# Weaving the next block's first products into the last steps of a block, in an attention and two-layer gated kernel on one Trainium2 core

## The chip, the cores and the metric

The kernel runs on one core of a Trainium2 chip. A core has TensorE (PE in the profile, with its weight loads as PEld), VectorE (DVE), ScalarE (ACT), GpSimd (POOL) and SyncE (SP, which issues the DMAs). The metric is the device time of one execution in microseconds, lower is better. Inputs and outputs lie in HBM in fp32; a difference in time of about 0.5% is what a measurement of this kernel can tell from no change.

## The reference

Pooled attention is followed by two gated two-matrix layers over the same 4608 tokens of width 512, with 2048 hidden features.

```python
def _attn_ref(q, k, v):                       # q, k, v: (8, 8, 576, 64)
    k_p = k.reshape(B, H, Sp, 8, D).mean(axis=3)
    v_p = v.reshape(B, H, Sp, 8, D).mean(axis=3)
    scores = scale * np.matmul(q, k_p.transpose(0, 1, 3, 2))
    scores = scores - np.max(scores, axis=-1, keepdims=True)
    attn = np.exp(scores)
    attn = attn / (np.sum(attn, axis=-1, keepdims=True) + 1e-09)
    return np.matmul(attn, v_p)

def _moe_ref(x, w_in, w_out):                 # layer 1
    h = x @ w_in
    g = np.where(h >= 1, h, np.where(h <= -1, 0.0, (h + 1) ** 2 / 4.0))
    return g @ w_out

def _moe2_ref(x, w_in, w_out):                # layer 2
    h = x @ w_in
    g = h - np.tanh(h)
    return g @ w_out
```

## The kernel before, in words

Everything is kept feature-major: a tile holds 128 features on its partitions and tokens along its columns. Layer 1 works through 16 blocks of 288 tokens (blk 0 to 15, two per batch entry), layer 2 through 9 blocks of 512 tokens. The attention of the next block runs inside the current layer 1 block. Every operand of TensorE is split in two (hi and lo, fp32r), and each product is the sum of three: hi times hi, hi times lo, lo times hi.

A block has FT = 16 hidden tiles of 128 features. For hidden tile j:

- `first_product(j)` on TensorE is 4 x 3 = 12 matmuls into one PSUM bank, the bank that `h_bank(j)` names. Its end increments `h_done`.
- In layer 1 the gate is a chain of five instructions: `clip` (DVE, L822), `bend` (ACT, the square, L678), `gate1` (DVE, maximum, L828), `round_gate` (ACT, g_hi, L687) and `split_gate` (DVE, g_lo, L815), which increments `g_split`. In layer 2 there is no clip: `bend` is a tanh from PSUM (L682), then `gate2` (L834), `round_gate` (L689), `split_gate` (L812).
- `second_product(j)` on TensorE is again 12 matmuls, three into each of the four banks of `acc_ps`, which are summed over the 16 tiles. The last one into each bank increments `acc_done`.

PSUM has eight banks of 512 fp32 columns: two in `h_ps`, `score_ps`, `att_ps`, and four in `acc_ps`. In layer 1 the first products alternate between the two banks of `h_ps`, but tile 2 goes into `att_ps`. In layer 2 four banks are used in turn.

The order of the work is written out by hand for each engine, as a loop over steps s = 0 to 15 of a block (`block_body`), and each engine runs its own list in order. On TensorE, step s is `second_product(s)`, then `first_product(s + 3)` as long as that tile is in the block (LAG = 3), with pieces of the next block's attention between them. So steps 13, 14 and 15 hold only second products. They are followed by the first products of tiles 0, 1 and 2 of the next block (written f0', f1', f2' below), and then by a wait for the sums to be read out of `acc_ps`, before second_product(0) of the next block may overwrite them.

DVE in step s does `split_gate` of tile s + 1 and then the clip and gate of tile s + 2; ACT does `round_gate` of tile s + 1 and `bend` of tile s + 2. The read-out, `copy_sums`, is two copies on ACT (L701, banks 0 and 2) and two on DVE (L842, banks 1 and 3); both engines have it in step 14, ahead of the clip or bend of tile 16, which is tile 0 of the next block.

DVE has work of the next batch entry too: `pool_k` (L853), the pooling of k, is one reduction in each of steps 11 to 14 of the blocks 0, 2, ... 12; sum_v, place_v and split_v stand in steps 0 to 7 of the blocks 1, 3, ... 13. Block 15 is the switch: its tiles are of layer 1, but f0', f1' and f2' after it are of layer 2, and the weights of layer 2 are loaded and split in it.

## Time and profile before

| | |
|---|---|
| median of 3 runs | 1795.99 us (1793.92 to 1802.9) |
| the profiled execution | 1793.92 us |
| its span, first to last instruction | 1792.0 us |
| PE busy | 1738.9 us (97%), 10480 matmuls |
| PEld busy | 1577.8 us (88%) |
| DVE busy | 874.3 us (49%) |
| ACT busy | 546.9 us (31%) |
| mean granted TensorE clock | 0.992 of full speed |
| chain that ended last | PE 85%, DVE 11%, ACT 2% |

The span is cut into two parts by the layers: up to about 985 us the layer 1 blocks, from there to the end the layer 2 blocks. In a timeline row the first number is the start in us, the second the duration in us, then engine, line, operation and tiles; a bracket holds the time for which the engine had been idle before the row, and what released it. Successive matmuls overlap in the pipeline, so the distance from one start to the next (0.13 us for 288 columns) is what a matmul costs, not its duration (0.29 us).

### The profile page before, as it was taken

What the parts mean: (1) busy time and instruction counts of PE and PEld (TensorE: products, weight loads), DVE (VectorE), ACT (ScalarE), POOL (GpSimd) and SP (SyncE); (2) the same over time, 40 slices, a digit from 0 to 9 for tenths busy, and PEclk for the clock granted to TensorE, in tenths of its full rate; (3) what the DMA queues carried; (4) which work ended last, traced back from release to release, by engine and by line L of the source; (5) the groups of instructions that cost most, each with busy time, mean ns of one, the idle gap of its engine ahead of it and who ended that gap; (6) DMA issues with size and microseconds to landing.
All of it is one profiled execution on the core that took longest, in us unless ns stands there. A gap on an engine that the chain in (4) does not pass through costs nothing.

```text
span 1792.0 us, 25053 instructions
## 1 busy us (share of the span) xinstructions
PE 1738.9 (97%) x10480; PEld 1577.8 (88%) x10480; DVE 874.3 (49%) x1745; ACT 546.9 (31%) x1141; POOL 160.2 (9%) x136
## 2 busy tenths in 40 slices
PE   4999999999999999999999999999999999999998
PEld 4999999999999999999999888888888888888887
DVE  6576676666856767668554222222222223232222
ACT  3533333333333333333335222222222222222221
POOL 4700011001000110011006100000000000000000
PEclk7999999999999999999999999999999999999999
DMA  5421012011110120111023101010101010000000
GB/s 163 153 63 64 15 39 77 26 30 61 39 64 16 37 78 26 58 34 39 14 71 132 60 0 48 0 47 0 47 5 42 9 38 15 32 18 29 23 1 24
DMA packets 47608, 77.81 MB, mean 43 GB/s; under 512 B 3488, under 2 KB 19872, under 8 KB 47520
## 3 DMA queue, kind: packets, MB, share of 16 engines
q1 hardware_dynamic: 47520, 76.56, 13.0%
q8 instruction: 64, 1.05, 0.2%
q14 instruction: 24, 0.20, 0.0%
HBM read 57.67 MB, written 18.87 MB: 43 GB/s over the span
## 4 chain that ended last, share of the span: by engine, by line
PE 85%; DVE 11%; ACT 2%; issue 0%; POOL 0%; DMA 0%; DVEq 0%; SPq 0%
PE acc_ps L502 40%; PE h_ps L492 29%; PE att_ps L492 6%; PE score_ps L492 6%; PE score_ps L517 2%; DVE k_diag L853 2%; DVE g_lo L815 1%; DVE v_sum L864 1%; DVE h_ps L828 1%; DVE bent L822 1%; PE score_ps L537 1%; ACT bent L678 1%; PE att_ps L529 1%; DVE v_tail L886 1%; DVE row_sum L907 1%; DVE prob L900 1%
## 5 line engine op out<-in xcount | busy, mean ns | idle before, releaser
L502 PE MATMUL acc_ps<-g_hi,wout_hi 128*128 128x288 f32 (+1 forms) x1600 | 541.0, 338 | 10.5 <-DVE g_lo L815 10.5
L502 PE MATMUL acc_ps<-g_hi,wout_lo 128*128 128x288 f32 (+1 forms) x1600 | 529.2, 331 | 0.0
L502 PE MATMUL acc_ps<-g_lo,wout_hi 128*128 128x288 f32 (+1 forms) x1600 | 528.9, 331 | 0.0
L492 PE MATMUL h_ps<-x_hi,win_hi 128*128 128x288 f32 (+1 forms) x1248 | 405.0, 325 | 15.0 <-DVE g_lo L815 9.6
L492 PE MATMUL h_ps<-x_hi,win_lo 128*128 128x288 f32 (+1 forms) x1248 | 398.6, 319 | 0.0
L492 PE MATMUL h_ps<-x_lo,win_hi 128*128 128x288 f32 (+1 forms) x1248 | 396.2, 317 | 0.0
L502 PEld LDWEIGHTS acc_ps<-g_hi,wout_hi 128*128 128x128 f32 x1600 | 302.6, 189 | 39.8 <-DVE g_lo L815 10.1
L502 PEld LDWEIGHTS acc_ps<-g_lo,wout_hi 128*128 128x128 f32 x1600 | 303.2, 190 | 25.3
L502 PEld LDWEIGHTS acc_ps<-g_hi,wout_lo 128*128 128x128 f32 x1600 | 302.4, 189 | 24.1
L492 PEld LDWEIGHTS h_ps<-x_hi,win_hi 128*128 128x128 f32 x1248 | 235.5, 189 | 31.5 <-DVE g_lo L815 13.6
L492 PEld LDWEIGHTS h_ps<-x_lo,win_hi 128*128 128x128 f32 x1248 | 237.1, 190 | 12.9
L492 PEld LDWEIGHTS h_ps<-x_hi,win_lo 128*128 128x128 f32 x1248 | 235.8, 189 | 12.8
L678 ACT ACTIVATE bent<-bent 128x288 f32<-128x288 f32 x256 | 113.9, 445 | 395.0 <-DVE bent L822 395.0
L815 DVE TENSOR_TENSOR g_lo<-h_ps,g_hi 128x288 fp32r<-128x288 f32 x240 | 109.3, 455 | 145.1 <-ACT g_hi L687 143.7
L834 DVE TENSOR_TENSOR h_ps<-h_ps,bent 128x512 f32<-128x512 f32 x72 | 50.4, 699 | 215.6 <-ACT bent L682 215.6
L828 DVE TENSOR_TENSOR h_ps<-h_ps,bent 128x288 f32<-128x288 f32 x240 | 110.6, 461 | 71.8 <-ACT bent L678 71.8
L822 DVE TENSOR_SCALAR bent<-h_ps 128x288 f32<-128x288 f32 x240 | 108.1, 450 | 59.6 <-PE h_ps L492 59.4
L682 ACT ACTIVATE bent<-h_ps 128x512 f32<-128x512 f32 x72 | 43.1, 599 | 227.8 <-PE h_ps L492 227.8
L687 ACT CAST g_hi<-h_ps 128x288 fp32r<-128x288 f32 x240 | 95.5, 398 | 39.2 <-DVE h_ps L828 39.2
L435 POOL TENSOR_TENSOR prob_tail<-prob,row_rcp 96x128 f32<-96x128 f32 x48 | 19.9, 415 | 754.4 <-DVE row_rcp L916 754.4
L834 DVE TENSOR_TENSOR att_ps<-att_ps,bent 128x512 f32<-128x512 f32 x36 | 25.2, 700 | 120.2 <-ACT bent L682 120.2
L492 PE MATMUL att_ps<-x_hi,win_lo 128*128 128x512 f32 (+1 forms) x208 | 76.1, 366 | 0.0
(125 smaller groups left out, 1825.1 us busy)
## 6 DMA issues: line engine op xcount, KB each, us to landing
stage<-kT SPq DMA_DIRECT2D x16, 576.0 KB, 5.2
q_sb<-qT SPq DMA_DIRECT2D x16, 576.0 KB, 3.9
x2T_scratch<-prob SPq DMA_DIRECT2D x16, 576.0 KB, 3.7
x_lo<-x2T_scratch SPq DMA_DIRECT2D x9, 1024.0 KB, 7.0
yT<-out_sb SPq DMA_DIRECT2D x9, 1024.0 KB, 5.0
stage<-v SPq DMA_DIRECT2D x8, 1024.0 KB, 8.3
stage<-w_in SPq DMA_DIRECT2D x8, 1024.0 KB, 5.0
stage<-w_out SPq DMA_DIRECT2D x8, 1024.0 KB, 5.3
```

Source lines behind the costliest of these rows:

```text
L435: nc.gpsimd.tensor_tensor(prob_tail[0:CH, c].rearrange("p (i a r) -> p i a r", i=2, a=PAIRS), tails.unsqueeze(1).to_broadcast(shape), seco ...
L492: last = nc.tensor.matmul(h_bank(j, layer)[:, 0:WIDTH[layer]], w[:, c, j * P:(j + 1) * P], x[:, c, 0:WIDTH[layer]], start=(c == 0 and i == ...
L502: last = nc.tensor.matmul(acc_ps[:, m, 0:WIDTH[layer]], w[:, j, m * P:(m + 1) * P], g[:, j % GRING, 0:WIDTH[layer]], start=(j == 0 and i = ...
L517: last = nc.tensor.matmul(bank[0:CH, e * 2 * KEYS:(e + 1) * 2 * KEYS], q_sb[:, p, c * CH:(c + 1) * CH], k_diag[:, p, :], start=True, stop= ...
L678: nc.scalar.activation(bent[:, j % 2, :], bent[:, j % 2, :], ACT.Square, bias=0.5, scale=0.5).then_inc(bent_done, 1)
L682: nc.scalar.activation(bent2[:, j % 2, :], h_bank(j, 2)[:, 0:T2], ACT.Tanh).then_inc(bent_done, 1)
L687: nc.scalar.copy(g_hi[:, j % GRING, :], h_bank(j, 1)[:, 0:T]).then_inc(g_hi_done, 1)
L815: nc.vector.tensor_tensor(g_lo[:, j % GRING, :], h_bank(j, 1)[:, 0:T], g_hi[:, j % GRING, :].bitcast(F32), ALU.subtract).then_inc(g_split, 1)
L822: nc.vector.tensor_scalar(bent[:, j % 2, :], h_bank(j, 1)[:, 0:T], 1.0, -1.0, ALU.min, ALU.max).then_inc(clip_done, 1)
L828: nc.vector.tensor_tensor(h, h, bent[:, j % 2, :], ALU.max).then_inc(gate_done, 1)
L834: nc.vector.tensor_tensor(h, h, bent2[:, j % 2, :], ALU.subtract).then_inc(gate_done, 1)
L853: last = nc.vector.tensor_reduce(k_diag[rows, cs, e * KEYS:(e + 1) * KEYS], kr[rows, cs], AX_X, ALU.add)
```

## The change

The first products of the next block are no longer issued in a row behind step 15: TensorE now issues f0' in step 13, f1' in step 14 and f2' in step 15, each behind that step's second product. The waits that stood ahead of f0' (for the next block's x, and at the switch for its weights) stand in step 13. Layer 1 uses the two banks of `h_ps` alone, so a first product of tile j waits until the tile before the last has left its bank (`g_split`); in the program's start f2' waits for tile 0 so. The read-out of the sums moves on both engines: on DVE from step 14 to step 15, behind the split of tile 16 and ahead of the clip of tile 17; on ACT to the end of the block, behind the bend of tile 17.

```diff
--- before.py
+++ after.py
@@ -258,10 +258,7 @@
 
         def h_bank(j, layer):
 
-            banks = [h_ps[:, 0], h_ps[:, 1], score_ps, att_ps]
-            if layer == 2:
-                return banks[j % 4]
-            return att_ps if j == 2 else banks[j % 2 if j < 2 else (j + 1) % 2]
+            return [h_ps[:, 0], h_ps[:, 1], score_ps, att_ps][j % (2 if layer == 1 else 4)]
 
 
         SWITCH_STEPS = {4 * q + 1: 2 * q for q in range(WCH)}
@@ -599,32 +596,30 @@
                             pe.wait_ge(k_pooled, att_b + 1)
                         attention(att, s, late=False, v_b=att_b)
                     j = s + LAG
-                    if j < FT:
-                        if first and j % WCH == 0:
+                    if j < FT or not last:
+                        nxt = j >= FT
+                        if s == FT - LAG:
+
+                            if att is not None:
+                                pe.wait_ge(x1_split, PAIRS * (att + 1))
+                            else:
+                                pe.wait_ge(x2_split, 2 * (blk + 2 - BLOCKS))
+                            if switch:
+
+                                pe.wait_ge(w_split, NW + 1)
+                        if first and j < FT and j % WCH == 0:
 
                             pe.wait_ge(w_split, 2 * (j // WCH) + 1)
                         if layer == 2 and j == FT - WCH:
 
                             pe.wait_ge(w_split, 2 * NW - 1)
-                        if layer == 2 and j >= 4:
-                            pe.wait_ge(g_split, t0 + j - 3)
-                        if layer == 1 and j >= 5:
-                            pe.wait_ge(g_split, t0 + j - 1)
-                        first_product(j, par, layer)
+
+                        pe.wait_ge(g_split, t0 + j - 3 if layer == 2 or (switch and j >= FT + 2) else t0 + j - 1)
+                        first_product(j % FT, (0 if switch else 1 - par) if nxt else par, 2 if switch and nxt else layer)
                     if att is not None:
                         attention(att, s, late=True, v_b=att_b)
 
                 if not last:
-
-                    if att is not None:
-                        pe.wait_ge(x1_split, PAIRS * (att + 1))
-                    else:
-                        pe.wait_ge(x2_split, 2 * (blk + 2 - BLOCKS))
-                    if switch:
-
-                        pe.wait_ge(w_split, NW + 1)
-                    for j in range(LAG):
-                        first_product(j, 0 if switch else 1 - par, 2 if switch else layer)
                     pe.wait_ge(acc_read_act, 2 * blk + 2)
                     pe.wait_ge(acc_read_dve, 2 * blk + 2)
 
@@ -652,6 +647,8 @@
             pe.wait_ge(x1_split, PAIRS)
             pe.wait_ge(w_split, 1)
             for j in range(LAG):
+                if j >= 2:
+                    pe.wait_ge(g_split, j - 1)
                 first_product(j, 0)
 
             block_body(0, 0, 1, att=1, first=True)
@@ -753,8 +750,6 @@
                     if s + 1 < FT or not last:
                         round_gate(t0 + s + 1, (s + 1) % FT, 2 if switch and s + 1 >= FT else layer)
                     j = s + 2
-                    if j == FT:
-                        copy_sums(blk, layer)
                     if j < FT or not last:
                         bend(t0 + j, j % FT, 2 if switch and j >= FT else layer)
                     if att is not None:
@@ -767,6 +762,7 @@
                         round_w(2, SWITCH_STEPS[s])
                     if first and s in FIRST_STEPS:
                         round_w(1, FIRST_STEPS[s])
+                copy_sums(blk, layer)
                 if switch:
 
                     act.wait_ge(acc_done, KT * (blk + 1))
@@ -981,11 +977,11 @@
                 for s in range(FT):
                     if s + 1 < FT or not last:
                         split_gate(t0 + s + 1, (s + 1) % FT, 2 if switch and s + 1 >= FT else layer)
+                    if s == FT - 1:
+                        copy_sums(blk, layer)
                     if att is not None:
                         attention(att, s, 1 - par, 0)
                     j = s + 2
-                    if j == FT:
-                        copy_sums(blk, layer)
                     if j < FT or not last:
                         if (layer == 2) or (switch and j >= FT):
                             gate2(t0 + j, j % FT)
```

The lists below are the first block (blk 0), an even one with `pool_k`. `g_lo`, `bent`, `h_ps` are split, clip and gate of one tile; the line numbers of the changed kernel are 3 or 4 lower.

DVE before, from the split of tile 15 on:

```order
122 L815 TENSOR_TENSOR g_lo<-h_ps,g_hi 128x288 [waits g_hi_done]
123 L842 COPY prob<-acc_ps 128x288 [waits acc_done,out_stored]
124 L842 COPY prob<-acc_ps 128x288 [waits acc_done]
125 L822 TENSOR_SCALAR bent<-h_ps 128x288 [waits h_done]
126 L828 TENSOR_TENSOR h_ps<-h_ps,bent 128x288 [waits bent_done]
127 L853 TENSOR_REDUCE k_diag<-stage 64x2x72
128 L815 TENSOR_TENSOR g_lo<-h_ps,g_hi 128x288 [waits g_hi_done]
129 L822 TENSOR_SCALAR bent<-h_ps 128x288 [waits h_done]
```

DVE now, from the same split on:

```order
122 L811 TENSOR_TENSOR g_lo<-h_ps,g_hi 128x288 [waits g_hi_done]
123 L818 TENSOR_SCALAR bent<-h_ps 128x288 [waits h_done]
124 L824 TENSOR_TENSOR h_ps<-h_ps,bent 128x288 [waits bent_done]
125 L849 TENSOR_REDUCE k_diag<-stage 64x2x72
126 L811 TENSOR_TENSOR g_lo<-h_ps,g_hi 128x288 [waits g_hi_done]
127 L838 COPY prob<-acc_ps 128x288 [waits acc_done,out_stored]
128 L838 COPY prob<-acc_ps 128x288 [waits acc_done]
129 L818 TENSOR_SCALAR bent<-h_ps 128x288 [waits h_done]
```

The two copies moved four instructions down: they stand behind the whole gate chain of tile 16 and ahead of the clip of tile 17.

ACT before, at the same place, from the rounding of tile 14 on (`g_hi` is round_gate, `bent` is bend):

```order
65 L687 CAST g_hi<-h_ps 128x288 [waits gate_done]
66 L678 ACTIVATE bent<-bent 128x288 [waits clip_done]
67 L687 CAST g_hi<-h_ps 128x288 [waits gate_done]
68 L701 COPY prob<-acc_ps 128x288 [waits acc_done,out_stored]
69 L701 COPY prob<-acc_ps 128x288 [waits acc_done]
70 L678 ACTIVATE bent<-bent 128x288 [waits clip_done]
```

ACT now, from the same instruction on:

```order
65 L684 CAST g_hi<-h_ps 128x288 [waits gate_done]
66 L675 ACTIVATE bent<-bent 128x288 [waits clip_done]
67 L684 CAST g_hi<-h_ps 128x288 [waits gate_done]
68 L675 ACTIVATE bent<-bent 128x288 [waits clip_done]
69 L684 CAST g_hi<-h_ps 128x288 [waits gate_done]
70 L675 ACTIVATE bent<-bent 128x288 [waits clip_done]
71 L698 COPY prob<-acc_ps 128x288 [waits acc_done,out_stored]
72 L698 COPY prob<-acc_ps 128x288 [waits acc_done]
```

The copies moved behind the bend of tile 17 (number 70), which waits for the clip of tile 17, number 129 of DVE's list.

## Rows read from the trace of the kernel before

**Rows 1.** Waits of PE: who waited for whom, total, times, longest.
```profile
PE acc_ps L502 <- DVE g_lo L815: 10.5, 15, 1.1
```

**Rows 2.** Windows, blocks 1 and 2: stretch, its length, busy PE, PEld, DVE, ACT, POOL, PEclk.
```profile
104.00:222.00 118.00, 115.38 (x877) 114.40 (x876) 79.74 (x178) 40.09 (x100) 9.81 (x12) 1.00 0.14 45
```

**Rows 3.** Timeline of PE, end of block 1: second products 13 and next 0.
```profile
156.98 0.29 PE L502 MATMUL acc_ps<-g_hi,wout_hi 128*128 128x288 f32 x1
...
166.51 0.29 PE L502 MATMUL acc_ps<-g_hi,wout_hi 128*128 128x288 f32 x1
```

**Rows 4.** Timeline of PE, end of block 2: second products 13, 15, next 0.
```profile
214.33 0.29 PE L502 MATMUL acc_ps<-g_hi,wout_hi 128*128 128x288 f32 x1
...
218.91 0.40 PE L502 MATMUL acc_ps<-g_hi,wout_hi 128*128 128x288 f32 x1 [1.08 <-DVE g_lo L815]
...
225.84 0.38 PE L502 MATMUL acc_ps<-g_hi,wout_hi 128*128 128x288 f32 x1 [0.32 <-DVE g_lo L815]
```

**Rows 5.** Timeline of DVE, end of block 2.
```profile
217.16 1.33 DVE L853 TENSOR_REDUCE k_diag<-stage 64x144 f32<-64x1152 f32 x1
218.42 0.44 DVE L815 TENSOR_TENSOR g_lo<-h_ps,g_hi 128x288 fp32r<-128x288 f32 x1
...
220.80 0.46 DVE L842 COPY prob<-acc_ps 128x288 f32<-128x288 f32 x1 [0.26 <-PE acc_ps L502]
222.39 0.46 DVE L822 TENSOR_SCALAR bent<-h_ps 128x288 f32<-128x288 f32 x1 [1.13 <-PE h_ps L492]
223.36 0.47 DVE L828 TENSOR_TENSOR h_ps<-h_ps,bent 128x288 f32<-128x288 f32 x1 [0.51 <-ACT bent L678]
223.85 1.35 DVE L853 TENSOR_REDUCE k_diag<-stage 64x144 f32<-64x1152 f32 x1
225.24 0.46 DVE L815 TENSOR_TENSOR g_lo<-h_ps,g_hi 128x288 fp32r<-128x288 f32 x1
```

**Rows 6.** Timeline of ACT, end of block 2.
```profile
212.76 0.45 ACT L678 ACTIVATE bent<-bent 128x288 f32<-128x288 f32 x1 [1.25 <-DVE bent L822]
213.11 0.39 ACT L718 ACTIVATE x_hi<-att_ps 128x288 fp32r<-128x288 f32 x1
...
220.40 0.40 ACT L701 COPY prob<-acc_ps 128x288 f32<-128x288 f32 x1 [0.34 <-PE acc_ps L502]
222.88 0.45 ACT L678 ACTIVATE bent<-bent 128x288 f32<-128x288 f32 x1 [2.08 <-DVE bent L822]
```

**Rows 7.** Timeline of DVE and PE inside block 3 (an odd one).
```profile
240.30 0.46 DVE L822 TENSOR_SCALAR bent<-h_ps 128x288 f32<-128x288 f32 x1 [0.51 <-PE h_ps L492]
...
257.79 0.40 PE L492 MATMUL h_ps<-x_hi,win_hi 128*128 128x288 f32 x1 [1.09 <-DVE g_lo L815]
```

**Rows 8.** Timeline of PE, DVE and ACT at the start of block 0.
```profile
41.03 0.29 PE L492 MATMUL att_ps<-x_hi,win_hi 128*128 128x288 f32 x1
51.57 0.40 PE L492 MATMUL h_ps<-x_hi,win_hi 128*128 128x288 f32 x1 [3.54 <-POOL win_lo L448]
...
41.54 0.46 DVE L815 TENSOR_TENSOR g_lo<-h_ps,g_hi 128x288 fp32r<-128x288 f32 x1 [0.47 <-ACT g_hi L687]
44.18 0.45 DVE L822 TENSOR_SCALAR bent<-att_ps 128x288 f32<-128x288 f32 x1
...
45.02 1.89 ACT L693 CAST win_hi<-stage 128x2048 fp32r<-128x2048 f32 x1
```

**Rows 9.** Timeline of PE in block 15, the switch.
```profile
970.20 0.40 PE L492 MATMUL h_ps<-x_hi,win_hi 128*128 128x288 f32 x1 [1.94 <-DVE g_lo L815]
...
971.98 0.44 PE L492 MATMUL h_ps<-x_lo,win_hi 128*128 128x288 f32 x1
...
979.80 0.29 PE L502 MATMUL acc_ps<-g_hi,wout_hi 128*128 128x288 f32 x1
...
993.85 0.39 PE L502 MATMUL acc_ps<-g_hi,wout_hi 128*128 128x512 f32 x1
```

**Rows 10.** Chain that ended last, at a layer 2 boundary: start, length, what.
```profile
1066.31 8.34 PE acc_ps L502 x36
```

## The prediction

> **What bounds the kernel now.** I read the page first: PE is busy 97% of the span and carries 85% of the chain that ended last. So the change can only win what PE idles, and only where it touches. The waits of PE come next: at second products PE waited for DVE's g_lo 15 times in layer 1, 10.5 us in all [rows 1]. The timeline at two block ends shows where. With P the time of one product of 288 columns, the end of block 1 (odd, no pooling of k) takes 166.51 - 156.98 = 9.53 us from second product 13 to the next block's second product 0 [rows 3]. That is six products without a gap, so P = 1.59 us. The end of block 2 (even, with pool_k) takes 225.84 - 214.33 = 11.51 us for the same six [rows 4]: 1.98 us lost, plus 0.08 because the first matmul after such a wait runs on 0.21 instead of 0.13 us. The reader is to see in rows 4 and 5 that second product 15 starts 0.05 us after the split of tile 15, which had to queue on DVE behind a 1.33 us k reduction, and that next second product 0 starts 0.14 us after the split of tile 16 (225.24 + 0.46), again behind a reduction. The PE clock is full there (PEclk 1.00 [rows 2]). In layer 2 three products take 8.34 us, P2 = 2.78, without a wait [rows 10].
>
> The two waits of an even block end, 1.08 and 0.32 us, come seven times (blocks 0, 2, ... 12) and make 9.8 of the 10.5 us. The other is 0.7 us at the switch.
>
> **Even block ends: what goes.** The new order gives every step two products, 3.18 us, where steps 13 to 15 had one, 1.59 us. Replaying block 2's rows: tile 15's split ends at 218.42 + 0.44 = 218.86. Until second product 13 nothing moves, so f0' starts behind it at about 216.0 (0.1 late: it waits for tile 14's split, as second product 14 did), then second product 14 at 217.6, and f1' at 219.2, the first to need that split: 0.4 us to spare. Second product 15 starts at 220.8, far later. Tile 16: f0' ends at 217.7; clip right behind tile 15's split at about 218.8; gate at +0.97 (222.39 to 223.36 in [rows 5]); then pool_k, 1.35; split of tile 16 at about 221.4 to 221.9. f2' wants it at 222.4. So both waits go, with 0.4 us to spare each. Only about 0.16 us (the 0.05 us gap at second product 14 and its slow first matmul) stays.
>
> **What comes: the wait for the sums.** Before, three first products (3P = 4.8 us) lay between the last second product and the overwriting of acc_ps; now one does, 1.59 us. Count from the start of second product 15, S. It ends at S + 1.59. DVE's second copy starts 0.20 us after that (second product 15 of block 2 ends at 218.91 + 1.69 = 220.60, copy at 220.80 [rows 5]), at S + 1.79. Clip of tile 17 is behind it; two instructions on DVE follow each other 0.08 us before the first one's end, so it starts at S + 2.17, though f1' had ended before S. Bend starts 0.49 later (222.39 to 222.88 [rows 5, 6]): S + 2.66. ACT's two copies are behind that bend: starts at +0.35 (212.76 to 213.11 [rows 6]), S + 3.01, and, overlapping by the same 0.08, 0.32 on, S + 3.33; with 0.40 each [rows 6] the last ends at S + 3.73. PE restarts 0.05 to 0.14 us later, S + 3.84, where f2' had ended at S + 3.18. So 0.66 us is idle and 0.11 lost in the first matmul: **0.77 us**, at each of the 15 block ends of layer 1 ahead of the switch, with or without pool_k. Bounds: at least the 0.3 us that is left if clip needed no place behind the copy's end and PE restarted at once; at most 1.3, if nothing overlapped (0.46 + 0.46 + 0.45 + 2 x 0.40 plus five hand-overs).
>
> Is something later late as well? Tile 17's rounding is behind the copies, S + 3.64, its split ends at S + 4.5; the next block's f3' needs it at S + 5.5. A margin of 1.0. Later in odd blocks DVE's sums of v build a queue, but it has drained by 240.30, where DVE waits for PE [rows 7]; so the 1.09 us wait at 257.79, 17 us on, behind place_v and split_v, stays as it is.
>
> **The start.** f2 now needs bank 0 back, so the split of tile 0, at 41.54 + 0.46 = 42.0, where it began at 41.03: 1.1 us later. Clip of tile 2 was not before 44.18 anyway, as it is behind tile 1's split on DVE; f2 now ends at about 43.8, so clip, bend and the 1.89 us weight rounding at 45.02 stay, and with them POOL's split that PE waits for until 51.57 [rows 8]. The 3.54 us wait covers the delay: 0. If the cover were gone it would cost 1.1 us once.
>
> **The switch.** From 979.80 to 993.85 are 14.05 us [rows 9] for three products of layer 1 and three of layer 2, 3 x 1.59 + 3 x 2.78 = 13.11: 0.94 lost before. Now f0' and f1' of layer 2 give second product 15 5.6 us more until it needs its split, and the bend of tile 17 there needs no clip and can run before the sums are complete, so the copies (0.40 and 0.46 us [rows 5, 6]) fit under the 2.78 us of f2'. Gain 0.9.
>
> **Layer 2.** No wait before, and one first product of 2.78 us covers the copies of 512 columns (by columns, 512/288 of 0.46, at most 0.82 us each), with no clip in the way of a bend: 0. The last block is unchanged.
>
> **Sum.** Seven even ends: 7 x (0.16 + 0.77 - 2.06) = -7.9 us. Eight others (1, 3, ... 13 and 14): 8 x 0.77 = +6.2. Switch -0.9. Total -2.6 us. The profiled execution took 1793.92 us (1.92 around its span); it would be 1791.3. It lies 2.1 us under the median, 1795.99, which would become 1793.4; I say 1793.
>
> **Rivals.**
> A, the forecast: the new wait eats most of the gain. 0.78.
> B, the sums are no wait: the copies end within f2'. Then only the gains are left, 7 x (2.06 - 0.16) + 0.9 = 14.2: 1782. For it: the copies are only 0.4 us each and PE's waits before name acc reads nowhere. Against: before they had 4.8 us of cover, and the order on ACT leaves them behind clip and bend. 0.06.
> C, slower: the new wait is at its upper bound, 1.3 us plus 0.1, and all 15 ends have it, 21 us against the 14.2 won. +7: 1803. It decides from where the wait passes 0.95 us per end. For it: ends 1, 3, ... had no loss at all before, so every one of the eight can only get worse. Against: the hand-overs are read from rows, and all of them would have to be longer together. 0.13.
> D, the clock: PE gets 15 new short stops. After the 1.94 us wait at 970.20 the clock fell to the lower level, 1.2 GHz: matmuls 0.24 apart with 0.44 us each [rows 9]; about 14 of them, 14 x 0.11 = 1.5 us. If each of the 15 ends had it: 1791 + 22, less than 1820. Against: even block ends had 1.08 and 0.32 us within 7 us and kept 1.00 [rows 2]. 0.03.
> The Trainium skill (TensorE: Matmul & The Clock Gate, A second HAM failure mode: psum-queue depth-cycling) speaks for D: short idling between groups of matmuls, as banks are cycled, can make the clock swing between its levels. By that rule the change would be rival D; by rows 2 the trace so far does not agree for stops of this size.
>
> **How the numbers follow.** A's own range is 1793 with 0.3 to 1.1 per end, -7 to +5, so 1786 to 1798. To hold 8 in 10 it is stretched toward C and the spread of the runs (1793.92 to 1802.9): 1785 to 1801. Under B and a corner of A the time falls by over 0.5% (9 us, what a measurement can tell): 0.08. Slower by more than that: D and a part of C, 0.08. Same: 0.84.
>
> **What would show it.** Right: PE's wait for g_lo at second products shrinks from 10.5 to under 1 us; a new row appears, PE acc_ps waiting for ACT's copy, 15 times 0.6 to 0.7 us, about 10 us; ends 13 to next 0 take 10.2 to 10.3 us in odd and in even blocks alike; a pair of blocks takes 118.5 - 1.1 + 0.8 = about 118.1 us. Wrong: that new row is missing or over 14 us; f1' or f2' wait for g_lo in even blocks; PEclk below 1.00 between 104 and 930; the start shifts the 51.57 row by more than 0.3 us; any new wait in layer 2.

## The result and the profile after

The changed kernel takes 1813.24 us (median of 6 runs, 1811.37 to 1814.03), the kernel before 1797.88 us (6 runs beside them, 1791.49 to 1805.08): ratio 1.0083, 95% interval 1.0055 to 1.011. It is slower by 0.8%, 20 us above the forecast and outside the range. The profiled execution took 1808.79 us with a span of 1806.9; 14.9 us more than the span of before. The six other runs of the changed kernel took 2.6 to 5.2 us more than this execution, at a granted clock of 0.988 or 0.989 in place of its 0.991; the profile doesn't show that part.

| stretch of the span (from the starts of PE's second product 0) | before | after | difference |
|---|---|---|---|
| up to block 0 | 42.62 | 42.25 | -0.4 |
| block 0, with the program's start in it | 64.74 | 60.81 | -3.9 |
| blocks 1 to 14 | 827.33 | 825.55 | -1.8 |
| block 15, the switch | 59.16 | 61.28 | +2.1 |
| layer 2, to the end of the span | 798.15 | 817.0 | **+18.9** |

The loss lies in the part for which the prediction said 0. PE's waits of the changed kernel (who waited for whom, total, times, longest) show three rows that answer to [rows 1]:

```profile
PE h_ps L489 <- DVE g_lo L811: 13.1, 10, 2.7
PE acc_ps L499 <- issue: 10.5, 5, 2.6
...
PE acc_ps L499 <- ACT prob L698: 5.8, 15, 0.4
PE acc_ps L499 <- DVE g_lo L808: 2.7, 1, 2.7
```

Second products no longer wait for g_lo in layer 1 (10.5 us before); they wait 15 times for ACT's copy of the sums, as forecast, 0.39 us each. What wasn't forecast: five waits at second products that end with "issue", nothing that the profile shows, and one of 2.7 us put down to a split of layer 2. All six lie in layer 2, two at each of three places, 1170, 1356 and 1540 us. There PE is at the first second product behind a return of the layer 2 loop (the branch at the end of its body, back to its start); the body holds two blocks. PE at the first of them:

```profile
1167.61 0.40 PE L489 MATMUL score_ps<-x_hi,win_lo 128*128 128x512 f32 x1
1170.48 0.49 PE L499 MATMUL acc_ps<-g_hi,wout_hi 128*128 128x512 f32 x1 [2.47 <-issue]
1170.81 0.39 PE L499 MATMUL acc_ps<-g_lo,wout_hi 128*128 128x512 f32 x1
...
1172.04 0.63 PE L499 MATMUL acc_ps<-g_hi,wout_hi 128*128 128x512 f32 x1
1172.47 0.63 PE L499 MATMUL acc_ps<-g_lo,wout_hi 128*128 128x512 f32 x1
1175.72 0.59 PE L499 MATMUL acc_ps<-g_hi,wout_lo 128*128 128x512 f32 x1 [2.63 <-issue]
...
1178.24 0.60 PE L489 MATMUL att_ps<-x_hi,win_lo 128*128 128x512 f32 x1
1178.67 0.41 PE L489 MATMUL att_ps<-x_hi,win_hi 128*128 128x512 f32 x1
```

PE stops, issues eight matmuls, and stops again, in the middle of a product. No wait of the program stands at the second place. Behind these stops matmuls of 512 columns are 0.43 us apart in place of 0.23: the lower clock, 1.2 of 2.4 GHz. There are 21 slow rows at the three returns. The six stops are 13.2 us, the slow matmuls 21 x 0.20 = 4.2, together 17.4 of the 18.9 us. The windows (stretch, length, busy PE, PEld, DVE, ACT, POOL, PEclk, DMA share, GB/s) of an undisturbed block and of the one behind a return:

```profile
1079.00:1168.00 89.00, 89.00 (x385) 71.79 (x383) 25.83 (x36) 21.82 (x36) 0.00 (x0) 1.00 0.07 25
1168.00:1264.00 96.00, 90.91 (x385) 73.29 (x384) 25.54 (x36) 21.81 (x36) 0.00 (x0) 0.96 0.06 21
```

Same number of matmuls, 89 us in the one and 96 in the other. The kernel before has no such stretch; there the same 96 us hold 416 matmuls:

```profile
1168.00:1264.00 96.00, 96.00 (x416) 77.86 (x415) 29.39 (x41) 24.60 (x41) 0.00 (x0) 1.00 0.10 35
```

The queues' part of the page gives the hint at the cause. Instruction packets of the changed kernel:

```profile
q8 instruction: 91, 1.49, 0.3%
```

and of the kernel before:

```profile
q8 instruction: 64, 1.05, 0.2%
```

Between 1150 and 1700 us the trace has none of them before, and 27 after: nine to each return, one about 6 us ahead of the branch (at 1160.2, 1345.3 and 1529.9 us) and eight behind it, the first of these at 1167.8, 1352.6 and 1536.6 us. One carries 16 KB (1.49 MB / 91). So PE's code of the loop is fetched again at each return. The record of the branch in the trace says so too: it takes 0.21 to 0.24 us at the three returns before, and 4.02, 3.89 and 4.38 us after. The loop's body has the same work in another order: the program differs in the number of instructions that it executes by 31 (25053 and 25084), and in where the loop lies.

### The profile page after: what moved, and what is told of

It reads as the page before. It is cut to its first block, busy times and chain, and to the rows that moved or that the text cites. A ratio compares the mean times of both kernels' runs of the same rounds, so it can differ in the third digit from the quotient of the medians.

```text
span 1806.9 us, 25084 instructions
## 1 busy us (share of the span) xinstructions
PE 1742.9 (96%) x10480; PEld 1577.5 (87%) x10480; DVE 876.2 (48%) x1745; ACT 543.6 (30%) x1141; POOL 160.2 (9%) x136
## 3 DMA queue, kind: packets, MB, share of 16 engines
q8 instruction: 91, 1.49, 0.3%
## 4 chain that ended last, share of the span: by engine, by line
PE 87%; DVE 8%; ACT 2%; issue 1%; DMA 1%; POOL 0%; SPq 0%; DVEq 0%
PE acc_ps L499 41%; PE h_ps L489 30%; PE att_ps L489 6%; PE score_ps L489 6%; PE score_ps L514 2%; DVE v_sum L860 1%; PE score_ps L534 1%; DVE bent L818 1%; DVE g_lo L811 1%; PE att_ps L526 1%; DVE v_tail L882 1%; DVE h_ps L824 1%; DVE row_sum L903 1%; DVE prob L896 1%; ACT prob L698 1%
## 5 line engine op out<-in xcount | busy, mean ns | idle before, releaser
L499 PE MATMUL acc_ps<-g_hi,wout_hi 128*128 128x288 f32 (+1 forms) x1600 | 541.5, 338 | 13.2 <-ACT prob L698 5.8
L489 PE MATMUL h_ps<-x_hi,win_hi 128*128 128x288 f32 (+1 forms) x1312 | 424.3, 323 | 17.2 <-DVE g_lo L811 13.1
L489 PE MATMUL h_ps<-x_hi,win_lo 128*128 128x288 f32 (+1 forms) x1312 | 417.2, 318 | 0.0
L489 PE MATMUL h_ps<-x_lo,win_hi 128*128 128x288 f32 (+1 forms) x1312 | 414.6, 316 | 0.0
L489 PEld LDWEIGHTS h_ps<-x_hi,win_hi 128*128 128x128 f32 x1312 | 247.3, 188 | 35.4 <-DVE g_lo L811 17.5
L489 PEld LDWEIGHTS h_ps<-x_lo,win_hi 128*128 128x128 f32 x1312 | 248.8, 190 | 12.9
L489 PEld LDWEIGHTS h_ps<-x_hi,win_lo 128*128 128x128 f32 x1312 | 247.5, 189 | 12.9
L811 DVE TENSOR_TENSOR g_lo<-h_ps,g_hi 128x288 fp32r<-128x288 f32 x256 | 116.6, 456 | 154.7 <-ACT g_hi L684 153.3
L824 DVE TENSOR_TENSOR h_ps<-h_ps,bent 128x288 f32<-128x288 f32 x256 | 118.1, 461 | 80.0 <-ACT bent L675 80.0
L818 DVE TENSOR_SCALAR bent<-h_ps 128x288 f32<-128x288 f32 x256 | 115.4, 451 | 58.1 <-PE h_ps L489 57.9
L830 DVE TENSOR_TENSOR score_ps<-score_ps,bent 128x512 f32<-128x512 f32 x36 | 25.2, 700 | 102.0 <-ACT bent L679 102.0
```

The source lines that it names most:

```text
L489: last = nc.tensor.matmul(h_bank(j, layer)[:, 0:WIDTH[layer]], w[:, c, j * P:(j + 1) * P], x[:, c, 0:WIDTH[layer]], start=(c == 0 and i == ...
L499: last = nc.tensor.matmul(acc_ps[:, m, 0:WIDTH[layer]], w[:, j, m * P:(m + 1) * P], g[:, j % GRING, 0:WIDTH[layer]], start=(j == 0 and i = ...
L811: nc.vector.tensor_tensor(g_lo[:, j % GRING, :], h_bank(j, 1)[:, 0:T], g_hi[:, j % GRING, :].bitcast(F32), ALU.subtract).then_inc(g_split, 1)
L818: nc.vector.tensor_scalar(bent[:, j % 2, :], h_bank(j, 1)[:, 0:T], 1.0, -1.0, ALU.min, ALU.max).then_inc(clip_done, 1)
L824: nc.vector.tensor_tensor(h, h, bent[:, j % 2, :], ALU.max).then_inc(gate_done, 1)
L830: nc.vector.tensor_tensor(h, h, bent2[:, j % 2, :], ALU.subtract).then_inc(gate_done, 1)
```

## The experiments

Each row below is one kernel; "layer 2" is the span less the start of second product 0 of block 16, of one profiled execution. The blocks there take 89.0 us in every kernel where no return disturbs them.

| kernel | median us (runs) | ratio to before, 95% | packets | block 16 at | layer 2 |
|---|---|---|---|---|---|
| before | 1797.88 (6) | | 64 | 993.85 | 798.2 |
| after | 1813.24 (6) | 1.0055 to 1.011 | 91 | 989.89 | 817.0 |
| wait_head | 1805.29 (6) | 1.0044 to 1.01 | 91 | 990.44 | 813.9 |
| layer1_only | 1802.88 (9) | 1.0041 to 1.0081 | 91 | 993.17 | 811.3 |
| quiet_boundary | 1800.2 (10) | 1.0006 to 1.0056 | 91 | 988.67 | 809.6 |
| before_pad23 | 1801.13 (10) | 1.0001 to 1.006 | 91 | 988.78 | 809.5 |
| after_pad96 | 1800.82 (10) | 1.0006 to 1.0057 | 65 | 1000.18 | 800.3 |
| unrolled | 1790.34 (10) | 0.9966 to 1.0002 | 82 | 989.39 | 798.0 |
| layer2_only | 1799.06 (10) | 0.998 to 1.0043 | 64 | 989.14 | 798.1 |
| before_noloop | 1790.38 (12) | 0.9983 to 1.0012 | 82 | 991.82 | 798.2 |
| act_first_noloop | 1779.51 (4) | 0.984 to 0.9947 | 82 | 980.48 | 798.0 |
| weights_early_noloop | 1786.13 (12) | 0.9946 to 0.9978 | 82 | 986.42 | 798.0 |
| act_first_weights_noloop | 1777.84 (6) | 0.9893 to 0.9939 | 82 | 980.31 | 798.0 |

The runs of before beside them had medians of 1797.9 to 1789.3 us, from 1788.8 to 1805.5 in all. So kernels are compared with each other by their profiles, and by medians where those lie close together in their own runs; medians that stand beside different runs of before can't tell 2 or 3 us from nothing.

**wait_head** is the changed kernel with the wait for the read-out of the sums moved from a block's end to the head of the next block, behind the return of the loop:

```diff
+                    if s == 0 and not first:
+                        pe.wait_ge(acc_read_act, 2 * blk)
+                        pe.wait_ge(acc_read_dve, 2 * blk)
...
-                if not last:
-                    pe.wait_ge(acc_read_act, 2 * blk + 2)
-                    pe.wait_ge(acc_read_dve, 2 * blk + 2)
```

> The changed kernel with one thing moved on PE: the wait for the sums to be read stands ahead of the next block's second product 0 (behind the loop's jump) instead of at the end of a block (ahead of the jump). Theory 1, jump: the 14.5 us of stops without a releaser at the three loop returns of layer 2, and the slow clock behind them, come because PE's sequencer stands at that wait right ahead of the jump, with only f2' (2.8 us) queued, so the code behind the jump is fetched too late. Then this kernel loses them: 1813 - 19 = about 1794, gaps at 1168 to 1176 gone. Theory 2, traffic: the fetch is slow because 2 MB of x2 and y move at that time; the jump comes earlier than the traffic here, so at least the second stop of each pair (2 to 3 us) stays: 1800 to 1808. Theory 3, it is not the code: no change, 1813.

The first stop of each pair went and the second grew to 3.01, 3.13 and 3.17 us, with 27 slow matmuls; the median, 1805.29, lies in the range of theory 2. The place of the wait shifts the loss, it doesn't make it.

**layer1_only** has the change in layer 1 and the switch; in layer 2 first products and copies stand as before (f0' to f2' in a row behind step 15, `copy_sums` in step 14).

> The changed kernel with layer 2 in its old order (three first products in a row behind step 15, read-out in step 14); layer 1 and the switch are as changed. If all of the loss lies at the loop returns (theory 1 or 2): 1813 - 19 = about 1794, that is the gain of layer 1 (6 us by the start of block 15) less the loss of the switch (2 us) against before, ratio about 0.998. If layer 1's 15 new waits cost more unprofiled than profiled: above 1800.

The time is 1802.88 us, not about 1794. The stops stay: 1.98 and 1.18 us, 2.08 and 0.81, 2.29 and 0.83, with 91 packets, though the order of layer 2's work is that of before. So the order of layer 2's work isn't what brings them.

**quiet_boundary** is the changed kernel with SP's output store and load of x at a boundary of layer 2 moved to the middle of a block:

```diff
+                sp.wait_ge(h_done, FT * 2 * b + FT + 8)
...
+                sp.wait_ge(h_done, FT * 2 * b + 2 * FT + 8)
```

> The changed kernel with the stores of y and the loads of x2 of layer 2 held back into the middle of the next block, so that no bulk transfer runs while PE returns in the loop. Theory 1: the first stop of each pair stays in part (the fetch itself is as long as before, 4.5 us from jump to first matmul against 1.9 us of cover), the total falls by what the traffic adds; 1805 to 1813. Theory 2: both stops go, 1794. In between: both theories hold a share, and the first stop's length tells the fetch time without traffic.

Stops and 91 packets stay, but five stops sum to 7.6 us instead of 13.2 for six, and layer 2 is 7.4 us shorter; the time, 1800.2, lies between the two theories. The store and the load don't cause the stops; they lengthen them. In the changed kernel the DMA engines are busy while the code is fetched: the first ten of these 40 slices of 1167 to 1190 us are over 0.9 full, up to 1172.8, past the first stop.

```profile
DMA  9999999999700000010000000000000000000000
GB/s 356 399 342 281 217 235 360 399 399 417 260 25 14 0 0 0 0 28 0 0 0 0 0 0 0 0 0 0 0 0 0 0 0 0 0 0 0 0 0 0
...
q1 hardware_dynamic: 1056, 2.10, 26.8%
q8 instruction: 3, 0.05, 0.9%
```

The trace shows how. With the quiet boundary the second code packet behind a return starts 0.5 to 0.6 us after PE has gone on; in the changed kernel, beside the store and the load, 2.2 to 3.1 us after (at the first return at 1173.3, with the last packet of the load ending at 1174.2).

**unrolled** is the changed kernel with the loop of layer 2 written out on SP, PE, ACT and DVE, with the same order of work:

```diff
-            with pe.Fori(BATCH, BATCH + BLOCKS2 // 2) as b:
+            for b in range(BATCH, BATCH + BLOCKS2 // 2):
```

> The changed kernel with the loop over pairs of layer 2 blocks written out in all engines, so there is no jump; the order of the work is the same. Theory 1: no stop at the three places, 1794. Theory 2 in its strong form (any fetch of code during traffic is slow): stops stay or spread, above 1800. Theory 3: 1813.

No stop is left in layer 2, the clock is full, every block takes 88.98 us, and the time falls from 1813.2 to 1790.3. The packets are 82, 19 of them between 1150 and 1700 us, and PE stops at none: it isn't the fetching that costs but a return to code that is gone.

**before_pad23** is the kernel before with 23 more semaphore instructions on PE ahead of the loop, each of which is already met, and nothing else:

```diff
+            for _ in range(45):
+                pe.wait_ge(w_split, 1)
```

> The kernel before, with 23 more semaphore instructions on PE ahead of the layer 2 loop, each of them satisfied at once; nothing else differs. They make PE's loop begin at its instruction 13873 instead of 13850, where it begins in the changed kernel. Theory 4, place: the stops come because the loop's code no longer stays with the engine but is fetched again at each return (instruction packets 91 instead of 64), and that depends on where the loop begins, not on the order of work. Then this kernel has 91 packets and three pairs of stops and takes 1794 + 10 to 19, so 1804 to 1813. Theory 1 (the wait in front of the jump with little queued) and theory 2 (traffic): 64 packets, no stop, 1794.

This is the experiment that names the cause. In the built program PE's loop begins at instruction 13850 before and at 13873 after, as the change adds 23 semaphore instructions ahead of it; the padding (two waits share an instruction) puts it at 13873 without moving any work. It has 91 packets, and PE's waits between 1079 and 1780 us are

```profile
PE acc_ps L502 <- issue: 8.7, 6, 2.3
```

where the kernel before has none. Layer 2 takes 11.3 us more than before. The DMA view of the same return, 1166 to 1189 us, in 40 slices, shows another difference from the changed kernel. The store and the load begin at 1160.4, ahead of the branch (1162.92), and the first code packet behind it starts as they end, at 1166.62. The branch takes 6.14 us, longer than in the changed kernel, but PE has three first products queued ahead of it, and they last 3.9 us past its start, where f2' alone lasts 1.6 us in the changed kernel: so the first stop is no longer than there, and the second fetch finds the DMA engines idle.

```profile
DMA  7100001000000100000000000000000000000000
GB/s 306 29 0 0 0 0 28 0 0 0 0 0 0 28 0 0 0 0 0 0 0 0 0 0 0 0 0 0 0 0 0 0 0 0 0 0 0 0 0 0
```

**after_pad96** is the changed kernel with 96 such instructions ahead of the loop, which then begins at 13969.

> The changed kernel with 96 satisfied semaphore instructions on PE ahead of the loop, so that it begins at 13969. Theory 4, if it goes by the offset within blocks of 16 KB (256 instructions): the loop covers 6.2 blocks, begins 0.57 into one and so touches seven, as the kernel before does if its real offset lies just under a border; 64 packets and 1790 as without a loop. Theory 4, if the place counts in another way (a limit on the whole program, say): 91 packets and 1811. Theory 1: no change, 1813.

The packets are 65 and the returns cost nothing (89.0 us a block). The padding itself has its price, once, ahead of block 16:

```profile
992.59 0.40 PE L489 MATMUL score_ps<-x_hi,win_lo 128*128 128x512 f32 x1
1000.18 0.79 PE L499 MATMUL acc_ps<-g_hi,wout_hi 128*128 128x512 f32 x1 [7.19 <-issue]
```

7.2 us and 11 slow matmuls. "issue" here is the padding itself: in the trace its 96 instructions run from 989.26 to 999.72 us, one each 0.106 us, and the matmuls queued ahead of them last until about 993. The 23 of before_pad23 take 2.4 us, up to 987.0, and are over before the queued matmuls are (988.8): no stop. Without its padding's price after_pad96 would be about where the unrolled kernel is.

**layer2_only** is the kernel before with the change in layer 2 alone. Its loop begins at 13850.

> The kernel before with the change in layer 2 alone: its loop begins at 13850, as before, and is 1582 instructions long, as changed (1580 before). Theory 4 by place: 64 packets, no stops, 1794 (layer 2 had no wait to win). Theory 4 by length, or theory 1 or 2: 91 packets and the stops, 1808 to 1813.

64 packets, no stop, 88.99 us a block: in layer 2 the moved work is worth nothing either way, as the prediction had it.

**before_noloop** is the kernel before with the loop written out.

> The kernel before with the layer 2 loop written out on all four engines; order of the work as before. Theory (place of the loop code): its layer 2 blocks take 89.0 us each with no stop at a return, as in the one profile of before, so nothing is gained there in a fetch-free execution: 1788 to 1792 us, and its runs lie within 5 us of each other, where those of before spread over 16 us, because there is no return whose code can be fetched again. If that holds, the change without the loop (1790.3) against this kernel is what the moved work alone is worth: within 2 us of zero. Rival (the spread of before has nothing to do with the loop): the runs spread over 10 us or more here too. Rival (the moved work itself costs the time): this kernel lies 10 us or more below the changed kernel without the loop, at 1780.

1790.38 us, from 1789.14 to 1795.03. By the trace PE executes 21100 instructions here, none twice; before it is 21252, of which 3 x 1580 are repeats. So 4588 different ones more came with 18 packets more (82 for 64), 255 to a packet: queue 8 carries PE's code.

The changed kernel without a loop has 1790.34, in runs of another occasion. By these medians the moved work alone is worth 0; by the two profiles (spans of 1790.0 and 1787.4) it is -2.6, but block 0 alone differs by 2.7, and it differs as much among the kernels that have it in the order of before (62.0 to 64.7). So it is worth somewhere between 0 and -3 us, and the -2.6 of the prediction is neither shown nor refuted.

The runs of this kernel spread over 5.9 us where those of before, beside them, spread over 12.4; that is the theory's side, though 5.9 is over the 5 it gave. In the table only the two kernels with the loop at 13850 have wide spreads (before, and layer2_only with 19.1 us; the others with a loop 2.7 to 6.4): a hint that the code is fetched there too in some executions, and not shown, as no trace caught one.

**act_first_noloop** is the unrolled kernel with ACT's copies ahead of the bend of tile 17 instead of behind it:

```diff
+                    if s == FT - 1:
+                        copy_sums(blk, layer)
...
-                copy_sums(blk, layer)
```

> The changed kernel without the loop (1790) and with ACT's two copies of the sums one place earlier, ahead of the bend of tile 17. My reckoning of the new wait has ACT's copies behind bend, clip and DVE's second copy as its only cause. Then the 15 waits for ACT (0.45 us each, 6.8 in all) go: 1790 - 7 = 1783. Rival: DVE's copy or the gate of tile 17 comes late in their place: 1788 to 1790.

1779.51 us. PE's wait for the copies is gone, as its rows at the end of block 2 show: the last first product and second product 0 of block 3 are 0.13 us apart.

```profile
220.44 0.29 PE L489 MATMUL h_ps<-x_hi,win_lo 128*128 128x288 f32 x1
220.57 0.29 PE L499 MATMUL acc_ps<-g_hi,wout_hi 128*128 128x288 f32 x1
```

Odd blocks take 59.06 us (59.73 in the unrolled kernel, 59.14 before), even ones 57.57 (58.24, 59.33).

**weights_early_noloop** is the unrolled kernel in which SP issues the first two weight loads of layer 2 ahead of the store of block 14's output:

```diff
+                if tail:
+                    sp.wait_ge(v_split, BATCH)
+                    load_w(2, 0)
+                    load_w(2, 1)
...
-                    sp.wait_ge(v_split, BATCH)
-                    load_w(2, 0)
-                    load_w(2, 1)
```

> The changed kernel without the loop, and on SP the loads of the first two layer 2 weight chunks stand ahead of the store of block 14's output instead of behind it. Theory (at the switch the weights are late because SP waits for the read-out of block 14's sums, which the change moved later): ACT's 3.7 us wait for the DMA in step 1 of block 15 goes, with PE's 2.1 to 2.7 us wait and the matmuls at the lower clock behind it; block 15 takes about 58 us in place of 61, and the time is 3 to 4 us below 1790.3, so 1786 to 1787.5. Rival (PE waits there because layer 1's bank rotation makes first products wait for the split, whatever the load does): ACT's wait goes but PE's 2 us stays, time unchanged within 1 us.

1786.13 us, 4.2 below the unrolled kernel; block 15 takes 56.8 us for 61.0, the same 4.2. ACT's wait for the DMA and PE's behind it are gone.

**act_first_weights_noloop** has both edits.

> The best version by the findings: the change, no loop, ACT's copies of the sums ahead of the bend of tile 17, and the first two layer 2 weight loads ahead of the store. Against 1779.5 of the version without the early weights: if the late weights cost 3 to 4 us at the switch, 1775.5 to 1777, and 1.1 to 1.3% below before. Rival (the two gains are one, since the earlier copies already let the store go earlier): 1779 to 1780, with ACT's DMA wait in block 15 already under 1 us in the version without early weights.

1777.84 us, 0.8% below before (0.9893 to 0.9939): the best version. It came 1.7 us below the one without early weights by medians of two occasions (2.1 in block 15 of the profiles, 58.2 for 60.3), not the 3 to 4 expected. There ACT's wait for the weights had been 2.8 us, already shorter than the 3.7 of the changed kernel, since the earlier copies let the store go earlier; the rival was half right.

**before_again** is the kernel before in one more profiled execution.

> The kernel before once more, one profiled look, to see what differs between its executions. Theory (the place of the loop code, met by chance): an execution near 1789 us has 64 packets on the instruction queue and no stop in layer 2; one at 1794 differs from it in the start alone, before 60 us; one at 1798 or more has 9 or 18 packets more and a stop of 2 us or more at one or two of the loop's returns. Rival: an execution at 1798 or more has 64 packets, and its loss lies elsewhere, as a lower clock or a late DMA.

1791.63 us with 64 packets and 798.1 us in layer 2, and it lies 2.3 us under the first profile of before by the start alone (block 16 at 991.56 for 993.85). So one execution of 1791 differs from one of 1794 ahead of layer 2. What the runs of 1798 and more have isn't settled, as no profile shows one.

## Why the prediction was wrong, step by step

**The step that failed is "Layer 2. No wait before, ... 0".** The work in layer 2 does behave so (layer2_only, unrolled). But the change adds 23 semaphore instructions to PE's program ahead of the layer 2 loop, and at the new place the loop's code no longer stays with the engine between two passes. That is shown from both sides: 23 instructions added to the kernel before bring 27 packets and six stops (before_pad23, +11.3 us in layer 2), 96 added to the changed kernel take them away (after_pad96), and so does writing out the loop (1813.2 to 1790.3). No rival of the prediction had this mechanism. Rival D comes to 1791 + 22 = 1813, the measured time to the microsecond, and that is chance: it had the lower clock behind the new waits of layer 1, where it stayed full. The slower side had 0.08. I had read the waits and the order of instructions, never their number between two places, nor the instruction queue's row.

The cost has two parts. With the order of before and the quiet boundary alike it is 11 to 12 us (809.5 and 809.6 for 798.2 us). In the changed kernel it is 18.9: there the second fetch meets the store of the output and the load of the next x, and a stop is 2.2 us on average in place of 1.5 (13.2 over six, 7.6 over five and 8.7 over six). They meet there because the change put the read-out of the sums later; with the order of before the first fetch meets them, under the cover of three first products. SP issues store and load before at

```profile
1164.52 0.40 SPq L324 DMA_DIRECT2D yT<-out_sb  x1
1165.56 0.38 SPq L317 DMA_DIRECT2D x_lo<-x2T_scratch  x1
```

7.4 us ahead of second product 0 (1171.88), and now at

```profile
1166.10 0.40 SPq L321 DMA_DIRECT2D yT<-out_sb  x1
1167.14 0.38 SPq L314 DMA_DIRECT2D x_lo<-x2T_scratch  x1
```

1.7 us ahead of the place where it was due (1167.84).

The Trainium skill (Runtime: NRT & Kernel Launch, Instruction fetch mechanics) says that engines get their code in blocks of 16 KB or 256 instructions, that TensorE's memory for it holds 2048, and that a taken branch whose target isn't in the current window of two blocks has to wait for a fetch. The trace agrees with the 16 KB of a packet and with the stall. It differs on the window: before, PE goes back 1580 instructions three times without a packet or a stop, and the measurement decides. By its words the rule stops both kernels alike; but it names the cost, and a rival in which it strikes one of them should have been there. By the page's figure, 256, a loop of 1580 instructions lies in seven or in eight blocks, depending on where it begins; the three places tried (13850 and 13969 without a stop, 13873 with) fit a reading in which eight are too many. Where the blocks begin was not measured, so that is an estimate and no finding: that the place decides is shown, the rule by which it does is open.

**The new wait, 0.77 us per end of a layer 1 block: right in kind, a little too large.** PE at the end of block 2, to hold against [rows 4]:

```profile
218.91 0.30 PE L489 MATMUL h_ps<-x_hi,win_hi 128*128 128x288 f32 x1
...
220.37 0.29 PE L489 MATMUL h_ps<-x_hi,win_lo 128*128 128x288 f32 x1
221.05 0.40 PE L499 MATMUL acc_ps<-g_hi,wout_hi 128*128 128x288 f32 x1 [0.39 <-ACT prob L698]
```

The start comes 0.68 us after the last row of f2', 0.55 more than the 0.13 of a running row, and 0.11 goes on its first matmul: 0.66. The profile's own count of the wait is 0.39 us, 5.8 in all, where the prediction named 0.6 to 0.7 and about 10 as its sign. DVE and ACT at the same place, to hold against [rows 5, 6]:

```profile
219.11 0.46 DVE L838 COPY prob<-acc_ps 128x288 f32<-128x288 f32 x1 [0.25 <-PE acc_ps L499]
219.48 0.45 DVE L818 TENSOR_SCALAR bent<-h_ps 128x288 f32<-128x288 f32 x1
```

```profile
219.96 0.45 ACT L675 ACTIVATE bent<-bent 128x288 f32<-128x288 f32 x1 [2.90 <-DVE bent L818]
220.31 0.68 ACT L698 COPY prob<-acc_ps 128x288 f32<-128x288 f32 x2
```

With S = 218.91 - 1.59 = 217.32 the copy starts at S + 1.79, the clip at S + 2.16, the bend at S + 2.64, the copies at S + 2.99: each within 0.02 us of the prediction's chain. Only the end is earlier, S + 3.67 (the two copies together are 0.68 us), and PE goes on 0.06 us behind it in place of 0.11. Odd blocks grew from 59.14 to 59.73 us, +0.6. That this wait is what the chain says, ACT's copies standing behind the bend, act_first_noloop shows: by medians of two occasions it takes 10.8 us off, and in the profiles blocks 1 to 15 take 10.0 us less.

**The even ends: right.** Both waits went; an even block takes 58.24 us for 59.33, -1.1 against 0.16 + 0.77 - 2.06 = -1.13. A pair of blocks takes 117.97 us, forecast 118.1. From second product 13 to the next 0 it is 10.29 us at even ends and 10.07 at odd ones (before: 11.51 and 9.52), forecast 10.2 to 10.3 at both. So two small errors offset each other at even ends: the new wait is 0.11 less than forecast, and of what was there 0.22 stays in place of 0.16. The wait in the middle of odd blocks stays, 1.10 for 1.09 in [rows 7]:

```profile
135.04 0.40 PE L489 MATMUL h_ps<-x_hi,win_hi 128*128 128x288 f32 x1 [1.10 <-DVE g_lo L811]
```

Blocks 1 to 14 together gave -1.8 us; the prediction's numbers for their ends make 8 x 0.77 - 6 x 1.13 = -0.6.

**The start, 0: can't be told from chance.** Block 0 took 60.8 to 62.8 us in the profiles with the changed order of layer 1 and 62.0 to 64.7 in those with the order of before; 1.1 us of the difference is its end, an even one. The wait for POOL's weight split is 2.28 us in the changed kernel, ended at 50.03, and 3.54 before [rows 8], but 2.3 in before_again too.

**The switch, -0.9: wrong, +2.1.** The loss at the end of block 15 went as said (13.12 us from second product 13 to the next 0, for 14.05), but one came at its start. The load of layer 2's first weights stands on SP behind the store of block 14's output, and that behind the read-out of its sums. Before, it was issued 3.6 us ahead of second product 0 of block 15 (934.69), now 0.4 behind it (928.61):

```profile
931.10 0.50 SPq L299 DMA_DIRECT2D stage<-w_in  x1
```

```profile
929.02 0.50 SPq L296 DMA_DIRECT2D stage<-w_in  x1
```

ACT in step 1 of block 15 and PE behind it:

```profile
936.79 1.90 ACT L690 CAST win_hi<-stage 128x2048 fp32r<-128x2048 f32 x1 [3.74 <-DMA stage<-w_in]
```

```profile
939.53 0.44 PE L489 MATMUL h_ps<-x_hi,win_hi 128*128 128x288 f32 x1 [2.70 <-DVE g_lo L811]
939.77 0.44 PE L489 MATMUL h_ps<-x_lo,win_hi 128*128 128x288 f32 x1
```

Before, ACT took up this cast at 939.36, with no wait. Now its data aren't there yet, 7.8 us after the issue, and round_gate, split and PE are queued behind it: 2.70 us, and 15 matmuls 0.24 apart in place of 0.13. The prediction had warned of nothing on SP: it followed PE, DVE and ACT through the switch and not the queue. Issuing the loads first took all of it away (4.2 us, weights_early_noloop). The +2.1 has luck in it: before, 13 matmuls of block 15 were slow behind the 1.94 us wait, and none after; against before_pad23 and layer2_only, where none was either (57.6 us for this block), the switch is 3.7 us longer.

**Rival D, the clock.** The Trainium skill (TensorE: Matmul & The Clock Gate, A second HAM failure mode: psum-queue depth-cycling) has short idling between groups of matmuls swing the clock. This case's trace doesn't agree for the stops of 0.39 and 1.10 us of layer 1: their window has the full clock, as [rows 2].

```profile
104.00:222.00 118.00, 116.01 (x880) 114.94 (x880) 80.24 (x179) 39.58 (x100) 9.80 (x12) 1.00 0.14 44
```

With longer ones it goes both ways. Behind 1.94 us at 970.20 it fell [rows 9], in before_again and before_noloop too; in before_pad23 and layer2_only it didn't, nor in the changed kernel behind the same wait:

```profile
968.72 0.40 PE L489 MATMUL h_ps<-x_hi,win_hi 128*128 128x288 f32 x1 [1.92 <-DVE g_lo L811]
968.96 0.30 PE L489 MATMUL h_ps<-x_lo,win_hi 128*128 128x288 f32 x1
```

**Where the gain went.** In the profiles the wins of layer 1 (1.8 us in blocks 1 to 14) and the loss at the switch (2.1) cancel; with the loop written out and ACT's copies and the weights put first, the gain is 12.5 us (1777.84 for the 1790.38 of before_noloop). The 18.9 us of the loop's code are more than the whole difference of the two profiles, 14.9.

## What to carry to other kernels

Where a kernel has a loop of well over a thousand instructions on an engine that is busy all the time, every edit ahead of it can move the loop to where its code is fetched anew at each return; count the packets of the instruction queue in both profiles before explaining a loss by the order of work, and test with a padding of idle waits or by writing the loop out. A read-out that is moved later takes with it what stands behind it on every queue, a DMA queue of another engine too. And a copy that frees a buffer for the bounding engine belongs ahead of an instruction that this engine doesn't need for several products: here that order alone was worth 0.7 us per block of layer 1.

## What the runs showed of the hardware that was not expected

- 23 met semaphore instructions on PE ahead of the loop cost 11.3 us in layer 2 (before_pad23); 96 ahead of the changed kernel's loop take its stops away, but cost 7.2 us at once (after_pad96). Such an instruction takes 0.106 us of PE's sequencer even when its wait is long met; the queued matmuls hid 23 of them and not 96.
- A return with fetching shows as nine packets of 16 KB, a branch of 3.4 to 6.2 us (0.2 without fetching) and, but for wait_head and one return of quiet_boundary, two stops of 0.4 to 2.7 us, eight matmuls apart.
- Code packets start late where data transfers run: 3.3 to 3.7 us behind the branch in before_pad23, as the store and the load end, and 1.1 to 1.3 us behind it in quiet_boundary.
- The clock fell behind some stops of 1.9 us and not behind others, never behind one of 1.1 us or less in blocks 1 to 14, and behind the first stop of all three pairs at the returns of the changed kernel. At the first return of quiet_boundary it stayed up behind 2.06 us, and at that of before_pad23 behind 2.28.
